# Moving two elementwise steps of a gated feed-forward stage from VectorE to GpSimd

## The reference

```
def _moe2_ref(x, w_in, w_out):          # x 2304x512, w_in 512x2048, w_out 2048x512
    h = x @ w_in
    sp = np.where(h > 20.0, h, np.log1p(np.exp(np.minimum(h, 20.0))))
    g = h * np.tanh(sp)
    return (g @ w_out).astype(np.float32)
```

## Time and profile before

| | us |
|---|---|
| runs | 801.52, 799.95, 800.55; median 800.55 |
| the profiled execution | 801.52 |
| its span, first to last instruction | 799.7 |
| mean granted TensorE clock | 0.991 of full |

### The profile page before, as it was taken

The page is one execution under the profiler, slowest core; times in us unless marked ns, Lnnn a source line. Parts: engine busy times, 40 slices in busy tenths (PEclk is TensorE's granted clock), DMA queues, the critical chain, the costliest instruction groups (busy, mean ns, idle before and its releaser), DMA issues.

```text
span 799.7 us, 13774 instructions
## 1 busy us (share of the span) xinstructions
PE 780.1 (98%) x4708; PEld 597.6 (75%) x4708; DVE 517.0 (65%) x1070; ACT 366.0 (46%) x881; POOL 110.8 (14%) x255
## 2 busy tenths in 40 slices
PE   8999999998999999998999999999999999999998
PEld 4788888878433333335889989889899899899896
DVE  3666666657011111154799888888888888888886
ACT  4666777730011011161465555555455455455454
POOL 3555555510201111100000000000000000000000
PEclk9999999997999999999999999999999999999999
DMA  5566888710577548002101010110101011001001
GB/s 204 168 183 171 286 281 272 235 35 9 214 274 289 207 180 302 15 20 95 43 1 41 1 40 1 40 41 1 41 0 39 0 39 39 0 0 38 3 1 41
DMA packets 50326, 77.79 MB, mean 97 GB/s; under 512 B 22083, under 2 KB 23363, under 8 KB 50240
## 3 DMA queue, kind: packets, MB, share of 16 engines
q1 hardware_dynamic: 48656, 72.19, 27.2%
q0 software_dynamic: 1600, 4.70, 1.6%
HBM read 65.36 MB, written 12.32 MB: 97 GB/s over the span
## 4 chain that ended last, share of the span: by engine, by line
PE 71%; DVE 3%; DMA 1%; issue 1%; ACT 1%; SPq 0%; POOLq 0%; POOL 0%; DVEq 0%
PE ps_y L1372 16%; PE ps_xt L1355 13%; PE ps_ht L1355 12%; PE ps_y L1062 9%; PE ps_h L1044 9%; PE ps_h L1372 8%; PE ps_h L1008 1%; DVE h_sb L952 1%; PE ps_ht L1051 1%; PE ps_h L1341 1%; DMA x_sb<-tokens 1%; DMA x_in<-tokens,job_entry 0%; PE ps_xt L1023 0%; PE ps_y L85 0%; DMA tokens<-y_sb,scatter_list 0%
## 5 line engine op out<-in xcount | busy, mean ns | idle before, releaser
L1244 ACT ACTIVATE u_sb<-u_sb 128x384 f32<-128x384 f32 x96 | 50.6, 527 | 105.9 <-DVE u_sb L1292 105.9
L1248 ACT ACTIVATE r_sb<-n_sb,all_consts 128x384 f32<-128x384 f32 x96 | 59.2, 617 | 85.3 <-DVE n_sb L1308 85.3
L367 ACT ACTIVATE probs<-ps_scores,neg_max 128x256 f32<-128x256 f32 (+2 forms) x160 | 66.7, 427 | 30.6 <-DVE neg_max L408 30.6
L1372 PE MATMUL ps_y<-ffn_lo,g_hi 128*128 128x512 f32 x192 | 76.6, 399 | 0.0
L1372 PE MATMUL ps_y<-ffn_hi,g_lo 128*128 128x512 f32 x192 | 76.0, 396 | 0.0
L1372 PE MATMUL ps_y<-ffn_hi,g_hi 128*128 128x512 f32 x192 | 75.8, 395 | 0.0
L408 DVE TENSOR_REDUCE neg_max<-ps_scores 128x2 f32<-128x512 f32 (+2 forms) x80 | 43.6, 578 | 37.4 <-PE ps_scores L507 36.7
L1355 PE MATMUL ps_xt<-xt_hi,ffn_lo 128*128 128x384 f32 x192 | 66.9, 348 | 0.8 <-DVE xt_lo L1283 0.8
L1355 PE MATMUL ps_ht<-xt_hi,ffn_lo 128*128 128x384 f32 x192 | 66.1, 344 | 0.0
L1320 DVE SCALAR_TENSOR_TENSOR u_sb<-n_sb,r_sb 128x384 f32<-128x384 f32 x96 | 53.7, 559 | 19.0 <-ACT r_sb L1250 19.0
L1355 PE MATMUL ps_xt<-xt_hi,ffn_hi 128*128 128x384 f32 x192 | 65.5, 341 | 0.0
(11 more groups left out here) (171 smaller groups left out, 1672.6 us busy)
## 6 DMA issues: line engine op xcount, KB each, us to landing
experts_even<-in_w SPq DMA_DIRECT2D x8, 2048.0 KB, 10.7
w_sb<-in_w SPq DMA_DIRECT2D x8, 2048.0 KB, 11.9
ffn_raw<-in_w_ffn SPq DMA_DIRECT2D x16, 512.0 KB, 5.7
q_raw<-in_qT SPq DMA_DIRECT2D x16, 288.0 KB, 3.7
k_raw<-in_kT SPq DMA_DIRECT2D x16, 288.0 KB, 4.6
v_sb<-in_v SPq DMA_DIRECT2D x16, 256.0 KB, 2.6
tokens<-x_out SPq DMA_DIRECT2D x64, 64.0 KB, 3.5
x_sb<-tokens SPq DMA_DIRECT2D x5, 768.0 KB, 4.6
```

The costliest lines, as they stand in the source:

```text
L367: e = nc.scalar.activation(probs[0:n, r, h, 0:w], ps_scores[t.ring][0:n, h, 0:w], ACT.Exp, bias=neg_max[0:n, r, h:h + 1], scale=-1.0, accu ...
L1244: nc.scalar.activation(u_sb[:, t.r], u_sb[:, t.r], ACT.Exp).then_inc(u_ready, 1)
L1248: nc.scalar.activation(r_sb[:, t.r], n_sb[:, t.f % NB], ACT.Ln, bias=cst["two"]).then_inc(ln_ready, 1)
L1372: m = nc.tensor.matmul(ps_o[i][:, :], a[:, t.r, P * i:P * i + P], ffn[b][:, at:at + D], start=(t.f == 0 and n == 0), stop=(t.f == FT - 1 a ...
```

## The change

The ratio (L1313) and g_lo (L1297) leave VectorE and become GpSimd instructions, in a new GpSimd program for this stage. VectorE's order in a step becomes L1292 (t), g (t2), a (t1), b (t1), n (t), and xt_lo of the transposes of the same step. ScalarE's order becomes Exp (t), g_hi (t2), the copies of a finished output, Ln and Exp (t), xt_hi. The pieces of the weights move to other steps. GpSimd alternates g_lo of a step with the ratio of the next. TensorE's and SyncE's programs stay as they are.

```diff
-    SPLIT = {f: n for n, f in enumerate((1, 2, 4, 5, 7, 8, 10, 11))}
+    SPLIT = {f: n for n, f in enumerate((1, 3, 4, 6, 7, 9, 10, 12))}
...
+    @block.gpsimd
+    def _(pool):
+        def ratio(s, f):
+            pool.wait_ge(b_ready, s + 1)
+            nc.gpsimd.tensor_tensor(n_sb[:, f % NB], n_sb[:, f % NB], r_sb[:, f % 2], ALU.mult).then_inc(ratio_ready, 1)
+
+        def low_part(s, f, later=True):
+            pool.wait_ge(g_hi_ready, s + 1)
+            if later:
+                pool.wait_ge(g_used, s - 1)
+            nc.gpsimd.tensor_tensor(g_lo[:, f % 2], n_sb[:, f % NB], g_hi[:, f % 2].bitcast(F32),
+                                    ALU.subtract).then_inc(g_lo_ready, 1)
+
+        last = CHUNKS * FT - 1
+        ratio(0, 0)
+        for f in range(NB - 1):
+            low_part(f, f, f >= 2)
+            ratio(f + 1, f + 1)
+        with pool.Fori(NB - 1, last, NB) as s:
+            for f in range(NB):
+                low_part(s + f, NB - 1 + f)
+                ratio(s + f + 1, NB + f)
+        low_part(last, last)
...
         def step(c, f, par):
-            t, t1, o = Step(c, f, 0, par), Step(c, f, 1, par), Step(c, f, LAG, par)
+            t, t2, o = Step(c, f, 0, par), Step(c, f, 2, par), Step(c, f, LAG, par)
             if t.exists():
                 act.wait_ge(min_ready, t.s + 1)
                 nc.scalar.activation(u_sb[:, t.r], u_sb[:, t.r], ACT.Exp).then_inc(u_ready, 1)
+            if t2.exists():
+                act.wait_ge(g_ready, t2.s + 1)
+                if t2.later(2):
+                    act.wait_ge(g_used, t2.s - 1)
+                    act.wait_ge(g_lo_ready, t2.s - 1)
+                nc.scalar.activation(g_hi[:, t2.r], n_sb[:, t2.f % NB], ACT.Copy).then_inc(g_hi_ready, 1)
+            if o.exists() and o.f == FT - 1:
... (the copies of a finished output, unchanged, now here)
+            if t.exists():
                 act.wait_ge(n_ready, t.s + 1)
... (Ln and Exp of r as before, then xt_hi; the old g_hi of t1 is gone)
             if t2.exists():
-                dve.wait_ge(g_hi_ready, t2.s + 1)
-                if t2.later(2):
-                    dve.wait_ge(g_used, t2.s - 1)
-                v.tensor_tensor(g_lo[:, t2.r], n_sb[:, t2.f % NB], g_hi[:, t2.r].bitcast(F32),
-                                ALU.subtract).then_inc(g_lo_ready, 1)
+                n = n_sb[:, t2.f % NB]
+                dve.wait_ge(ratio_ready, t2.s + 1)
+                v.scalar_tensor_tensor(out=n, in0=n, scalar=-1.0, in1=ps_h[t2.f % HB][:, 0:C], op0=ALU.mult,
+                                       op1=ALU.mult).then_inc(g_ready, 1)
             if t1.exists():
-                u, r = u_sb[:, t1.r], r_sb[:, t1.r]
+                u, n, r = u_sb[:, t1.r], n_sb[:, t1.f % NB], r_sb[:, t1.r]
+                dve.wait_ge(r_ready, t1.s + 1)
+                v.scalar_tensor_tensor(out=u, in0=n, scalar=2.0, in1=r, op0=ALU.add, op1=ALU.mult).then_inc(a_ready, 1)
                 dve.wait_ge(a_ready, t1.s + 1)
                 v.scalar_tensor_tensor(out=r, in0=u, scalar=2.0, in1=r, op0=ALU.subtract,
                                        op1=ALU.mult).then_inc(b_ready, 1)
... (n of t as before)
-            if t1.exists():
-                n, r = n_sb[:, t1.f % NB], r_sb[:, t1.r]
-                dve.wait_ge(b_ready, t1.s + 1)
-                v.tensor_tensor(n, n, r, ALU.mult).then_inc(ratio_ready, 1)
-                dve.wait_ge(ratio_ready, t1.s + 1)
-                v.scalar_tensor_tensor(out=n, in0=n, scalar=-1.0, in1=ps_h[t1.f % HB][:, 0:C], op0=ALU.mult,
-                                       op1=ALU.mult).then_inc(g_ready, 1)
-            if t.exists():
-                u, n, r = u_sb[:, t.r], n_sb[:, t.f % NB], r_sb[:, t.r]
-                dve.wait_ge(r_ready, t.s + 1)
-                v.scalar_tensor_tensor(out=u, in0=n, scalar=2.0, in1=r, op0=ALU.add, op1=ALU.mult).then_inc(a_ready, 1)
             ahead = next_chunk(c, par)
-            if f - 1 in AHEAD and ahead:
-                xt_part(*ahead, AHEAD[f - 1])
+            if f in AHEAD and ahead:
+                xt_part(*ahead, AHEAD[f])
```

More of the change, by code:

```diff
@@ L1244, in step @@
                 nc.scalar.activation(u_sb[:, t.r], u_sb[:, t.r], ACT.Exp).then_inc(u_ready, 1)
+            if t2.exists():
[5 more added lines that the diff above has]
+            if o.exists() and o.f == FT - 1:
+                for i in range(CT):
+                    act.wait_ge(*((o_ready, o.c * (CT - 1) + i + 1) if i < CT - 1 else (g_used, o.s + 1)))
+                    if i == 0 and (not isinstance(o.c, int) or o.c >= 1):
+                        act.wait_ge(o_stored, o.c * 16)
+                    nc.scalar.activation(o_sb[:, i], ps_o[i][:, :], ACT.Copy).then_inc(o_copied, 1)
+            if t.exists():
                 act.wait_ge(n_ready, t.s + 1)
```

## The result

The changed kernel takes 806.84 us (median of 9 runs, 804.73 to 811.32) against 800.03 for the kernel before (9 runs, 795.71 to 801.52). The ratio is 1.0097, 95% interval 1.0074 to 1.012: slower, by 5.9 to 9.6 us. The forecast was 807.0, so it was right; three of its four terms were not, as the trace shows.

What follows compares the result with a forecast made beforehand. TensorE, 98% busy, was taken as the bound. Start 0.5, chunk 0 3.2 and tail 2.8 sum to 6.5 us on the profiled 801.52, giving 808.0; less 0.97 for the median, 807.0, range 802.4 to 819.

Steps and rivals of the forecast that it cites:

- TensorE is the bound and the stage has 2.3 us to give: Feed-forward stage: TensorE, 98% busy, waits only 1.64 us before its first output matmul and 0.6 at the end.
- POOL's price 1.005 us: One 384-column ratio or g_lo instruction on GpSimd, scaled from 1415 ns at 576 columns plus a fixed part of some 0.19.
- Turns at the port, b undisturbed, n stretched to 1.3: VectorE instructions with two SBUF inputs and GpSimd's take turns, first come, first served; n goes from 0.55 to about 1.3 us.
- Start 0.5: First output matmul of the stage: the longer first g_lo chain costs 0.1 to 0.5 us, taken as 0.5.
- Chunk 0, 3.2 us: Chunk with weight pieces: three VectorE steps take 13.94 us against TensorE's 13.01, so TensorE waits 3.2 us in all.
- Middle nothing, with 0.16 us to spare: Chunks 1 to 5: transpose steps leave g_lo 0.16 us of cover, so TensorE narrowly waits for nothing.
- wrong if TensorE waits in the middle: Sign that would refute the forecast; it expected no TensorE waits for g_lo from 450 to 785 us.
- The rival with a slower GpSimd: At 1.1 us per GpSimd instruction TensorE waits in later transpose steps too: some 14 us, 815; chance 0.24.
- Tail 2.8: Last three output steps: longer chains through GpSimd start the last output 2.8 us later with turns, 2.1 without.
- Sum 6.5: Whole kernel: 0.5 at the first output, 3.2 in chunk 0 and 2.8 at the last outputs make 6.5 us slower.
- A slower GpSimd makes it worse from 1.05 us on: Middle of the stage: predicted cost some 14 us at 1.1 us per GpSimd instruction, 25 at 1.2, 60 at 1.415.
- the rival without collisions: Ports hardly collide: first output 0.1, chunk 0 nothing, last outputs 2.1; 2.3 us slower, 802.9; chance 0.17.

Runs made afterwards that it cites:

- the LAG 4 runs: Kernel before with TensorE using each tile one step later (LAG 4, not 3), four g_hi and g_lo buffers: ratios 0.9957 and 0.9956 to the kernel before.
- the run with n first: Changed kernel in which GpSimd's g_lo also waits for VectorE's n of the same step: ratio 1.0083 to the kernel before, +4.7 us at equal clock.

## Why the prediction was right, and where not

- *TensorE is the bound and the stage has 2.3 us to give.* Right; the LAG 4 runs took 3.0 (start distances count a little more than the brackets).
- *POOL's price 1.005 us.* 0.99 alone: right to 2%.
- *Turns at the port, b undisturbed, n stretched to 1.3.* Right: 0.56 and 1.35. n has the same tile as both inputs and counts as two. The Trainium skill (SBUF — State Buffer, "Who interferes with whom") names this contention for two SBUF inputs, under its rule of an exclusive lock; its words "for the whole instruction" stand beside VectorE's two-port modes. A lock on whole instructions would leave the waiter at some 1.0 + 0.55 us, an estimate, and n takes 1.35, so the measured form is nearer the cheaper one that the prediction took.
- *Start 0.5.* Measured 0.1; mis-sized, as g_lo got the port before n of step 2.
- *Chunk 0, 3.2 us: three steps of VectorE 13.94 against 13.01, three full groups and 0.3.* The mechanism is what the runs show (14.30 against 13.01, and TensorE's pace was VectorE's), but the term was mis-sized: 4 x 1.29 = 5.2. Each of the three steps was 0.1 us longer than worked out (5.45, 4.42, 4.43), and the first group pays in full. The 0.1 comes from the hand-overs: counted from the minimum, n ends at 3.33 us, the ratio at 4.21 and the piece at 4.49, where the working has 3.29, 4.12 and 4.38.
- *Middle nothing, with 0.16 us to spare.* The cover was just short: 1.0 us over 13 places of under 0.1. No bracket shows a wait there, but by its own sign, "wrong if TensorE waits in the middle", this term failed. The rival with a slower GpSimd had named the place.
- *Tail 2.8.* 2.9.
- *Sum 6.5.* 9.2 at equal clock, so the terms were 2.7 us short. That the measured median lies 0.2 us from the forecast is luck. The nine executions behind it had a mean clock of 0.996; the nine of before, whose clocks aren't on record, had by the line and their median some 0.992 (an estimate), and that difference hides 2.3 us of the cost. The interval of the ratio (5.9 to 9.6 us) holds both figures.
- *A slower GpSimd makes it worse from 1.05 us on.* Not so simple: one instruction more in GpSimd's queue made it better, as it changed who came first at the port. The prediction treated the turns' order as given. What a truly slower GpSimd instruction would do wasn't tried.
- Slips in the working, none above 0.15 us: a group of chunk 0 enters the sum with 0.97 where 13.94 - 13.01 is 0.93; 1.64 + 0.6 is 2.2 and not 2.3; the rival without collisions adds up to 2.2 and not 2.3; and the passage on the lock has 6.6 for the sum of 6.5.

## What to carry to other kernels

Before work is moved to GpSimd, list which VectorE instructions beside it have two SBUF inputs, and who asks for the port first in each step: the one with the longer chain behind it should, and one wait can decide that. Such a wait acts wherever it stands, at the ends of the pipeline too, where it cost 1.4 us here. A buffer more covers a late result but not an engine whose round is longer than the bound's, so compare rounds first (here 14.3 against 13.0 us), waits after. And look at the ends of a pipeline separately: there the whole latency of a chain is paid, which is where one step of lag was worth 3 us to the kernel before. And read the granted clock of each stretch before a difference of starts is called a wait.

## What the runs showed of the hardware

- Two engines at the port cost the waiter the other's reading, about 0.8 us of a 1.0 us GpSimd instruction (n 0.55 to 1.35, piece 0.42 to 1.23) and 0.3 us of VectorE's 0.55 (GpSimd 0.99 to 1.33); with one operand in PSUM n takes 0.547 and GpSimd's two 1.02 and 1.03.
- A GpSimd tensor_tensor on two columns took 0.20 us alone, like tensor_scalar on two (0.21), and 0.47 behind VectorE's b, so a tiny instruction takes its turn as well; on 384 columns it took 0.99 alone.
- The same program's span moves by 6.9 us with 0.01 of mean granted clock, more than most effects here. Lengths of the stage, or executions of equal clock, told +3.0 from +9.2 where two ratios of runs (1.0078 and 1.0097) could not.
- At a granted clock of 0.50 matmuls of 512 columns start 0.43 us apart instead of 0.23; one such stretch cost 1.4 to 1.5 us. In the profiles of four experiments it fell right behind TensorE's wait before the first output (2.53 us in the run with n first); that the wait is the cause wasn't tested.
